# Causal mask moved from TensorE products into decay rows made by GpSimd, and parts of x prepared two slots earlier

## The chip, the cores and the metric

One core of a Trainium2 chip runs the whole kernel. The metric is the device time of one execution in microseconds (us). The engines are TensorE (PE in the profile, with its weight loads as PEld), VectorE (DVE), ScalarE (ACT), GpSimd (POOL) and SyncE (SP), which issues all the DMAs here.

## What is computed

Causal attention with a decay term, then a gated MLP, then a soft mixture of experts with 8 small experts. Cut to the part that the change touches:

```python
# q, k, v: (4, 8, 576, 64); f: (4, 8, 576)
scores = scale * q @ k.T
cum    = cumsum(log(clip(f, 1e-4, 1)))              # per batch and head
decay  = cum[:, None] - cum[None, :]
scores = where(upper triangle, -1e9, scores + decay)
attn   = softmax(scores)                            # row by row
out    = attn @ v                                   # 576 x 64 for each of 32 heads
# the 8 heads of a batch side by side are x (576 x 512), the input of the MLP:
h = x @ w_in;  g = h * sigmoid(1.702 * h);  x2 = g @ w_out
# then slots = softmax over tokens, 8 experts on 32 slots, and a mix back to the tokens
```

## The kernel before

The 32 heads are processed in order, n = 8 b + s for batch b and head s. Each head has five query tiles i = 0 to 4 (128 rows each, 64 in the last), and tile i needs only the keys up to its own diagonal block, 128 i + 128 columns (576 for tile 4). The kernel keeps the scores negated: TensorE makes -scale q k in `yb`, VectorE adds the row `cum` of the keys and takes the minimum along the row (L824, one instruction a tile, with a second one that reads the minimum out), ScalarE takes exp with scale -1 and that minimum as bias (L689). The causal mask is a constant `mask` of 128 x 128 that holds 1e9 above the diagonal. Before the change it is added by a matmul, identity times `mask_r`, into the diagonal block of each tile (L1059): five matmuls a head, 160 in all. `cum` is a row of 576 numbers, copied to all 128 partitions by one DMA a head (`load_cum`, L530) into `cum_b`, two heads deep.

Operands are kept as a high and a low part (fp32r). So ScalarE makes high parts (`qs`, `kh`, `pth`, `xh`, `gh`, `wih`, `woh`), VectorE or GpSimd the low parts. GpSimd's part of a head is `vsplit` (L626, L628) and `dup` (L615, L617), which copies the key parts to the other half of the partitions; TensorE's next scores wait for it. For x, ScalarE copies `xh` (L713) and GpSimd subtracts to `xl` (L633) for the pairs of heads 0 to 2; for pair 3, finished last, VectorE makes `xl` (L855).

The order of all engines' work is written out by `batch_steps`, which each engine's block walks with its own name. A slot is the stretch in which head s is scored and head s - 1 is turned, multiplied with v and summed. Batch 0 runs its attention alone ("begin" branch, slots 0 to 8; TensorE does 16 constant products, `fill`, L1082, in each slot). In batches 1 to 3 each slot also holds nine gaps, f(), into which the 64 units of the MLP of the batch before are spread. A unit is 12 matmuls of 288 columns (L1204); units alternate between two banks of `mb`, and a unit waits until the bank's last unit has been read. Eight units of the first kind (h, tanh on ScalarE L736, product on VectorE L925) alternate with eight of the second (into `x2t`, VectorE L932). The weights come quarter by quarter through a two-deep `stage` (L497), split by ScalarE (L675) and GpSimd (L660); GpSimd also makes `gl` (L643).

In the steps of a slot, VectorE's softmax normalisation (`norm`: L831, L833 and L838, one instruction for each of tiles 0 to 3; tile 4's is ScalarE's, L696) is followed by the first score tile of the next head ("early"). In slot 8, where the batch's last head is finished, the parts of x follow: on ScalarE `norm`, three xh copies (`early_x`), `pv` (L707, out of the attention's product), the fourth xh copy; on VectorE the sum of `pv` (L850) and the fourth xl. The first unit of the MLP waits for all four.

## Time and profile before

| | |
|---|---|
| median of 3 runs | 759.37 us (758.19 to 760.92) |
| the profiled execution's own time | 759.59 us |
| its span, first to last instruction | 757.8 us |
| TensorE busy | 712.0 us, 94% of the span, 6027 matmuls |
| VectorE, ScalarE, GpSimd busy | 58%, 58%, 53% |
| mean granted TensorE clock | 0.989 |
| chain that ended last | TensorE 78%, VectorE 10%, ScalarE 8%, issue 2% |
| HBM traffic | 126 GB/s over the span |

The span has four parts: batch 0's attention alone up to about 97 us, batches 1 to 3 with the MLP between (to about 566 us), the last batch's MLP (to about 685 us), and the mixture of experts. A matmul's duration in a row is its latency; matmuls overlap, so what one costs is read from the distance between starts. Rows of the same line that follow each other are merged, with their count behind an x.

### The profile page before, as it was taken

The page shows a single profiled execution, that of the slowest core. Times are in us where ns is not written, and L with a number is a line of the kernel's source. Part 1 is how long each engine was busy: PE and PEld are TensorE (multiplying, and loading weights), DVE is VectorE, ACT ScalarE, POOL GpSimd, SP SyncE. Part 2 cuts the span into 40 slices and gives each one's busy share as a digit, 9 for nine tenths or more (in the row PEclk, how much of TensorE's full clock was granted, in tenths as well). Part 3 has the DMA queues.
Part 4 walks back from the last instruction along what each step waited for, and adds up shares of the span by engine and source line. Part 5 has one row for each costly group of instructions (what it writes and reads, how often), then busy time and mean ns, then how long its engine had stood idle before and what let it go on. Part 6 is the DMA issues. An engine that isn't in the chain of part 4 may idle for free.

```text
span 757.8 us, 15776 instructions
## 1 busy us (share of the span) xinstructions
PE 712.0 (94%) x6027; PEld 678.2 (90%) x6027; DVE 443.0 (58%) x1255; ACT 435.9 (58%) x1031; POOL 399.5 (53%) x439
## 2 busy tenths in 40 slices
PE   3999979999999999999999999999999999998993
PEld 3888879999999999999999999999999999995562
DVE  6898857676776656675666566766542332225323
ACT  4788867575757675666666675757564344321113
POOL 3355357474747755565757573848385476530000
PEclk9999989999999999999999999999999999999998
DMA  4433323333333333333331413332214445499976
GB/s 105 107 93 107 93 67 89 89 89 88 96 95 96 96 84 94 85 106 85 107 85 48 133 37 95 95 108 68 70 44 139 139 141 193 136 394 376 380 301 250
DMA packets 90362, 96.65 MB, mean 128 GB/s; under 512 B 61296, under 2 KB 61296, under 8 KB 88240
## 3 DMA queue, kind: packets, MB, share of 16 engines
q1 hardware_dynamic: 90288, 95.66, 40.5%
q8 instruction: 48, 0.79, 0.4%
q14 instruction: 26, 0.21, 0.1%
HBM read 90.84 MB, written 4.79 MB: 126 GB/s over the span
## 4 chain that ended last, share of the span: by engine, by line
PE 78%; DVE 10%; ACT 8%; issue 2%; DMA 0%; POOL 0%; SPq 0%; DVEq 0%; POOLq 0%
PE mb L1204 51%; PE yb L1057 6%; PE zb L1076 5%; PE xb L1103 5%; PE mb L1256 2%; ACT prob L689 2%; DVE prob L838 2%; PE xb L1037 2%; DVE ptl L844 1%; ACT xh L713 1%; PE yb L1295 1%; PE yb L1059 1%; DVE kl L806 1%; DVE qs L802 1%; ACT qs L681 1%
## 5 line engine op out<-in xcount | busy, mean ns | idle before, releaser
L1204 PE MATMUL mb<-xh,wih 128*128 128x288 f32 x512 | 158.8, 310 | 7.4 <-DVE xl L855 4.3
L1204 PE MATMUL mb<-gh,woh 128*128 128x288 f32 x512 | 156.8, 306 | 3.1 <-DVE x2t L932 3.0
L1204 PE MATMUL mb<-xl,wih 128*128 128x288 f32 x512 | 151.5, 296 | 0.0
L1204 PE MATMUL mb<-xh,wil 128*128 128x288 f32 x512 | 151.3, 296 | 0.0
L1204 PE MATMUL mb<-gl,woh 128*128 128x288 f32 x512 | 150.8, 294 | 0.0
L1204 PE MATMUL mb<-gh,wol 128*128 128x288 f32 x512 | 150.8, 294 | 0.0
L643 POOL TENSOR_TENSOR gl<-hid,gh 128x288 fp32r<-128x288 f32 x128 | 105.1, 826 | 70.4 <-ACT gh L730 68.8
L925 DVE SCALAR_TENSOR_TENSOR hid<-gate,mb 128x288 f32<-128x288 f32 x128 | 57.6, 451 | 113.9 <-ACT gate L736 113.4
L689 ACT ACTIVATE prob<-prob,m_row 64x576 f32<-64x576 f32 (+4 forms) x160 | 96.5, 604 | 35.1 <-DVE m_row L824 34.2
L660 POOL TENSOR_TENSOR wol<-stage,woh 128x512 fp32r<-128x512 f32 x64 | 82.9, 1295 | 62.9 <-ACT woh L675 62.8
L660 POOL TENSOR_TENSOR wil<-stage,wih 128x512 fp32r<-128x512 f32 x64 | 82.1, 1291 | 56.9 <-ACT wih L675 56.7
L1204 PEld LDWEIGHTS mb<-xh,wih 128*128 128x128 f32 x512 | 96.9, 189 | 10.2 <-DVE hid L925 4.8
L736 ACT ACTIVATE gate<-mb 128x288 f32<-128x288 f32 x128 | 52.5, 410 | 83.8 <-PE mb L1204 83.1
L1204 PEld LDWEIGHTS mb<-gh,woh 128*128 128x128 f32 x512 | 96.3, 188 | 4.4 <-DVE x2t L932 3.9
L1204 PEld LDWEIGHTS mb<-xl,wih 128*128 128x128 f32 x512 | 97.1, 190 | 0.0
L1204 PEld LDWEIGHTS mb<-xh,wil 128*128 128x128 f32 x512 | 96.7, 189 | 0.0
L1204 PEld LDWEIGHTS mb<-gl,woh 128*128 128x128 f32 x512 | 96.3, 188 | 0.0
L1204 PEld LDWEIGHTS mb<-gh,wol 128*128 128x128 f32 x512 | 96.0, 188 | 0.0
L824 DVE CUSTOM_DVE_ANT_0 prob<-yb,cum_b 64x576 f32<-64x576 f32 (+4 forms) x160 | 83.5, 537 | 10.4 <-issue 9.8
L844 DVE TENSOR_TENSOR ptl<-zb,pth 128x512 fp32r<-128x512 f32 (+1 forms) x128 | 73.1, 571 | 24.4 <-ACT pth L702 23.8
L702 ACT CAST pth<-zb 128x512 fp32r<-128x512 f32 (+1 forms) x128 | 62.9, 491 | 41.7 <-PE zb L1076 41.1
L932 DVE SCALAR_TENSOR_TENSOR x2t<-mb,x2t 128x288 f32<-128x288 f32 x96 | 43.4, 454 | 71.2 <-PE mb L1204 71.0
(196 smaller groups left out, 1464.6 us busy)
## 6 DMA issues: line engine op xcount, KB each, us to landing
stage<-in_moe_w_in SPq DMA_DIRECT2D x64, 256.0 KB, 3.0
stage<-in_moe_w_out SPq DMA_DIRECT2D x64, 256.0 KB, 2.6
ring_a<-in_moe_w SPq DMA_DIRECT2D x16, 1024.0 KB, 6.7
ring_b<-in_moe_w SPq DMA_DIRECT2D x14, 1024.0 KB, 11.8
cum_b<-cum_dram SPq DMA_DIRECT2D x32, 288.0 KB, 3.7
qk_in<-in_q SPq DMA_DIRECT2D x32, 144.0 KB, 3.0
qk_in<-in_k SPq DMA_DIRECT2D x32, 144.0 KB, 3.7
v_in<-in_v SPq DMA_DIRECT2D x32, 128.0 KB, 3.2
```

The source lines that it names most:

```text
L643: pool.tensor_tensor(gl[:, i % FT, HALF * (i // FT):HALF * (i // FT + 1)], hid[:, i % RING, :], gh[:, i % FT, HALF * (i // FT):HALF * (i / ...
L660: pool.tensor_tensor(lo[:, t, :], stage[:, t % 2, :], hi[:, t, :].bitcast(F32), ALU.subtract).then_inc(w_lo, 1)
L689: nc.scalar.activation(prob[0:r, par, POFF[i]:POFF[i] + w], prob[0:r, par, POFF[i]:POFF[i] + w], ACT.Exp, bias=m_row[0:r, par, i:i + 1], s ...
L702: nc.scalar.copy(pth[:, lo:hi], zb[:, c % 2, 0:hi - lo]).then_inc(p_hi, 1)
L736: nc.scalar.activation(gate[:, j % RING, :], bank_of("unit", m, u)[:, 0:HALF], ACT.Tanh, scale=GATE / 2).then_inc(h_tanh, 1)
L824: nc.vector.tensor_tensor_reduce(prob[0:r, par, o:o + w], ybf[0:r, base:base + w], cum_b[0:r, par, 0:w], 1.0, 3e38, ALU.add, ALU.min, m_ro ...
L844: nc.vector.tensor_tensor(ptl[:, lo:hi], zb[:, c % 2, 0:hi - lo], pth[:, lo:hi].bitcast(F32), ALU.subtract).then_inc(p_lo, 1)
L925: nc.vector.scalar_tensor_tensor(out=hid[:, j % RING, :], in0=gate[:, j % RING, :], scalar=1.0, in1=bank[:, 0:HALF], op0=ALU.add, op1=ALU. ...
L932: nc.vector.scalar_tensor_tensor(out=dst, in0=bank[:, 0:HALF], scalar=0.5, in1=dst, op0=ALU.mult, op1=ALU.add).then_inc(unit_out, 1)
L1057: mm(ybf[:, base + k0:base + k0 + kw], qs[:, par, P * i:P * i + P], x[:, par, k0:k0 + kw], start=not last, stop=last, skip_group_check=True)
L1076: ins = tr(zb[:, c % 2, at:at + P], prob[:, par, POFF[i] + P * kt:POFF[i] + P * kt + P], swapped if back else ident)
L1204: ins = mm(bank[:, 0:HALF], a[:, t, P * (j % 4):P * (j % 4) + P], x[:, t, cols], start=(i == 0), stop=(i == 11))
```

## The change

Four things:

1. For batches 1 to 3 the mask matmul is gone. The decay row is instead loaded once for each query tile (`COFF`: where each tile's copy begins in 1856 columns), so that each has a diagonal block of its own, and GpSimd adds `mask` to those blocks: 64 x 64 for tile 4 (`cmask_4`, behind `dup`), and two instructions of two 128 x 128 blocks each for the others (`cmask`). `cmask` waits for `normed`, VectorE's normalisation of the head before. Even heads use free space in `x2tok`, odd heads the place of the old `cum_b`.
2. SyncE issues five DMAs of cum a head instead of one; four of them (tiles 3, 2, 0, 1) go behind the loads of v, q and k of the same slot.
3. In batch 0 the parts of x's pairs 0 and 1 are made in slot 7, that of pair 2 in slot 8. On ScalarE pairs 0 and 2 stand at the slot's beginning and pair 1 ahead of `norm`; on GpSimd pairs 0 and 2 stand behind `vsplit` and pair 1 behind `cmask`. In later batches `early_x` is as it was.
4. TensorE does 16 constant products ahead of the first unit of batch 0's MLP.

```diff
+CW = 1856
+COFF = [512, 1024, 640, 0, 1280]
@@ batch_steps
         if engine == "pool":
-            qk, dup = qk + dup, []
+            qk, dup = qk + dup + following_head("cmask_4"), []
+            early = following_head("cmask")
@@
+        first_x = [[(1, ("xsplit", kt))] if begin and engine in ("act", "pool") and slot == at_slot else []
+                   for kt, at_slot in enumerate((HEADS - 1, HEADS - 1, HEADS))]
@@ begin branch
+            if engine == "act":
+                steps += first_x[0] + first_x[2]
@@
-                          + norm + early_x + pv + xs[3])
+                          + first_x[1] + norm + pv + xs[3])
             else:
-                steps += (vsplit + pt(0) + score(1) + pt(1) + score(2) + qk + pt(2) + score(3) + dup + pt(3)
-                          + norm + early + early_x + pv + xs[3])
+                steps += (vsplit + pt(0) + score(1) + first_x[0] + first_x[2] + pt(1) + score(2) + qk + pt(2) + score(3) + dup + pt(3)
+                          + norm + early + first_x[1] + pv + xs[3])
@@ SyncE, load_cum (first in a slot's load) and load_cum_tiles (last in it)
+                sp.dma_start(cum_t[s % 2][0:QW[4], COFF[4]:CW], cum_dram[bass.ds(n, 1), :].to_broadcast([QW[4], SEQ])
+                             ).then_inc(c_dma_4[s % 2], 16)
+                for i in (3, 2, 0, 1) if n >= HEADS else ():
+                    w = P * i + QW[i]
+                    sp.dma_start(cum_t[s % 2][:, COFF[i]:COFF[i] + w], cum_dram[bass.ds(n, 1), 0:w].to_broadcast([P, w])
+                                 ).then_inc(c_dma[s % 2], 16)
@@ GpSimd
+                elif st[0] == "cmask_4":
+                        pool.wait_ge(c_dma_4[n % 2], 16 * (n // 2 - 3))
+                        pool.tensor_tensor(at, at, mask[0:QW[4], 0:QW[4]], ALU.add).then_inc(c_masked_4, 1)
+                elif st[0] == "cmask":
+                        pool.wait_ge(c_dma[n % 2], cum_loaded(n))
+                        pool.wait_ge(normed, n)
+                        for at in (blocks[:, 0:5:4, :], blocks[:, 1:7:5, :]):
+                            pool.tensor_tensor(at, at, mask[:, :].unsqueeze(1).broadcast_to([P, 2, P]), ALU.add
+                                               ).then_inc(c_masked, 1)
@@ VectorE, score
+                        if b:
+                            dve.wait_ge(c_masked_4, b * 8 + s - HEADS + 1)
+                    elif g < 3 and b:
+                        dve.wait_ge(c_masked, 2 * (b * 8 + s - HEADS) + g)
@@ TensorE, score
-                        ins = mm(ybf[:, base + P * i:base + P * i + r], ident_r[:, :], mask_r[:, 0:r],
-                                 start=False, stop=True, skip_group_check=True)
+                        if b == 0:
+                            ins = mm(ybf[:, base + P * i:base + P * i + r], ident_r[:, :], mask_r[:, 0:r],
+                                     start=False, stop=True, skip_group_check=True)
@@ TensorE, unit
+                    if b == 1 and st[1] == 0 and m == 0:
+                        constant_products()
```

## Rows read from the trace of the kernel before

**Rows 1.** Windows view, busy time of each engine in the three middle batches

```profile
core 0: us, PE busy (x) PEld busy (x) DVE busy (x) ACT busy (x) POOL busy (x), PEclk, DMA share, GB/s
105.40:260.00 154.60, 150.92 (x1167) 149.10 (x1167) 106.44 (x285) 101.64 (x244) 99.49 (x108) 1.00 0.33 90
260.00:420.00 160.00, 157.92 (x1251) 155.53 (x1250) 101.61 (x296) 105.24 (x253) 99.47 (x109) 1.00 0.33 91
420.00:566.00 146.00, 145.27 (x1148) 142.98 (x1146) 88.06 (x254) 94.38 (x227) 87.58 (x94) 1.00 0.28 79
```

**Rows 2.** Chain that ended last, from 105 to 566 us, shares by line

```profile
by line: PE mb L1204 59.0%; PE yb L1057 8.2%; PE zb L1076 7.5%; PE xb L1103 7.3%; PE xb L1037 1.9%; ACT xh L713 1.6%; PE yb L1059 1.5%; DVE prob L838 1.3%; ACT gate L736 1.1%; issue 1.0%; ACT gh L730 1.0%; DVE hid L925 0.9%; ACT prob L689 0
```

**Rows 3.** Timeline of TensorE, matmuls with idle time before them: start, duration, [idle <-releaser]

```profile
101.02 0.61 PE L1204 MATMUL mb<-xh,wih 128*128 128x288 f32 x1 [4.28 <-DVE xl L855]
...
121.78 0.40 PE L1204 MATMUL mb<-xh,wih 128*128 128x288 f32 x1 [1.40 <-DVE hid L925]
...
153.73 0.40 PE L1204 MATMUL mb<-xh,wih 128*128 128x288 f32 x1 [0.83 <-DVE hid L925]
...
252.28 0.40 PE L1204 MATMUL mb<-gh,woh 128*128 128x288 f32 x1 [1.36 <-DVE x2t L932]
...
566.40 0.40 PE L1204 MATMUL mb<-gh,woh 128*128 128x288 f32 x1 [0.25 <-DVE x2t L932]
```

**Rows 4.** Timeline of TensorE: 16 constant products, and one mask matmul among scores

```profile
81.70 1.98 PE L1082 MATMUL mb<-mask_r,ident_r 128*128 128x128 f32 x16
...
298.64 0.22 PE L1059 MATMUL yb<-mask_r,ident_r 128*128 128x128 f32 x1
298.70 0.39 PE L1057 MATMUL yb<-kh,qs 128*128 128x384 f32 x1
298.93 0.34 PE L1057 MATMUL yb<-kl,qs 128*128 128x384 f32 x1
```

**Rows 5.** Timeline at the end of batch 0's last slot

```profile
94.15 0.37 PE L1057 MATMUL yb<-kh,qs 128*128 128x288 f32 x1
...
95.41 0.28 PE L1103 MATMUL xb<-ptl,vs 128*128 128x64 f32 x1
95.43 1.80 ACT L713 CAST xh<-xst 128x576 fp32r<-128x576 f32 x3
...
96.23 4.11 POOL L633 TENSOR_TENSOR xl<-xst,xh 128x576 fp32r<-128x576 f32 x3 [2.18 <-ACT xh L713]
...
97.26 0.63 ACT L707 COPY olow<-xb 64x576 f32<-64x576 f32 x1
...
99.41 1.55 DVE L855 TENSOR_TENSOR xl<-xst,xh 128x576 fp32r<-128x576 f32 x1 [0.74 <-ACT xh L713]
```

**Rows 6.** Timeline of the same slot: ScalarE at its beginning, GpSimd's dup

```profile
87.69 0.59 ACT L702 CAST pth<-zb 128x512 fp32r<-128x512 f32 x1 [0.26 <-PE zb L1076]
...
91.81 1.14 POOL L615 TENSOR_TENSOR kh<-kh,mask 64x576 fp32r<-64x576 f32 x1 [2.55 <-ACT kh L683]
```

**Rows 7.** Windows view behind TensorE's long idle time (columns as in rows 1)

```profile
103.00:105.00 2.00, 2.00 (x12) 1.99 (x10) 0.25 (x1) 0.70 (x2) 0.00 (x0) 0.50 0.00 0
```

**Rows 8.** Groups of instructions, GpSimd: busy us, mean ns of one

```profile
L643 POOL TENSOR_TENSOR gl<-hid,gh 128x288 fp32r<-128x288 f32 x128 | 105.1, 826 | 70.4 <-ACT gh L730 68.8
```

**Rows 9.** Groups of VectorE, one normalisation tile at 208.1 and at 94.5 us

```profile
L838 DVE TENSOR_SCALAR prob<-prob,rsum 128x384 f32<-128x384 f32 x1 | 1.4, 1443 | 0.0
...
L838 DVE TENSOR_SCALAR prob<-prob,rsum 128x384 f32<-128x384 f32 x1 | 0.4, 415 | 0.0
```

**Rows 10.** Timeline at the end of batch 1's last slot

```profile
246.99 4.20 POOL L633 TENSOR_TENSOR xl<-xst,xh 128x576 fp32r<-128x576 f32 x3 [1.71 <-ACT xh L713]
...
251.10 0.76 DVE L855 TENSOR_TENSOR xl<-xst,xh 128x576 fp32r<-128x576 f32 x1 [0.74 <-ACT xh L713]
...
251.78 0.81 DVE L932 SCALAR_TENSOR_TENSOR x2t<-mb,x2t 128x288 f32<-128x288 f32 x2
```

**Rows 11.** Timeline of SyncE's queue, the one cum load of a head

```profile
255.40 0.43 SPq L530 DMA_DIRECT2D cum_b<-cum_dram  x1
```

More of the change, by code:

```diff
@@ L292, in build @@
         v_in = sb("v_in", [P, 2, QT, DIM], F32, att_mem)
-        cum_b = sb("cum_b", [P, 2, SEQ], F32, att_mem)
+        cum_1 = sb("cum_1", [P, CW], F32, att_mem)
+        cum_b = cum_1[:, 0:2 * SEQ].rearrange("p (x n) -> p x n", x=2)
+        cum_t = (x2tok[:, 2 * QT:3 * QT, :].rearrange("p i n -> p (i n)")[:, 0:CW], cum_1[:, :])
         qs = sb("qs", [P, 2, QT * P], F32R, att_mem)
@@ L372, in build @@
         c_dma = [sem(f"c_dma{i}") for i in range(2)]
+        c_dma_4 = [sem(f"c_dma_4{i}") for i in range(2)]
+        c_masked = sem("c_masked")
+        c_masked_4 = sem("c_masked_4")
         w_dma = [sem(f"w_dma{i}") for i in range(2)]
@@ L463, in bank_of, with cum_loaded @@
             return mb[:, place[kind, m, i] % 2, :]
+        def cum_loaded(n):
+            return 16 * (n // 2 + 1) if n < HEADS else 64 + 16 * (QT - 1) * (n // 2 - 3)
         def is_last(m):
@@ L528, in load_cum, with load_cum_tiles @@
                 wait_from(sp, decayed, 5 * (n - 1))
-                src = cum_dram[bass.ds(n, 1), :].to_broadcast([P, SEQ])
-                sp.dma_start(cum_b[:, s % 2, :], src).then_inc(c_dma[s % 2], 16)
+                if n < HEADS:
+                    sp.dma_start(cum_b[:, s % 2, :], cum_dram[bass.ds(n, 1), :].to_broadcast([P, SEQ])
+                                 ).then_inc(c_dma[s % 2], 16)
+                    return
+                sp.dma_start(cum_t[s % 2][0:QW[4], COFF[4]:CW], cum_dram[bass.ds(n, 1), :].to_broadcast([QW[4], SEQ])
+                             ).then_inc(c_dma_4[s % 2], 16)
+            def load_cum_tiles(b, s):
+                n = b * 8 + s
+                for i in (3, 2, 0, 1) if n >= HEADS else ():
+                    w = P * i + QW[i]
+                    sp.dma_start(cum_t[s % 2][:, COFF[i]:COFF[i] + w], cum_dram[bass.ds(n, 1), 0:w].to_broadcast([P, w])
+                                 ).then_inc(c_dma[s % 2], 16)
             def step(b, m, st):
@@ L538, in step @@
                         load_qk((n + 1) // HEADS, (n + 1) % HEADS)
+                    load_cum_tiles(b, st[1])
                 elif st[0] == "weights":
@@ L618, in step @@
                     pool.wait_ge(k_dup, 2 * n + 2)
+                elif st[0] == "cmask_4":
+                    n = b * 8 + st[1]
+                    if n >= HEADS:
+                        pool.wait_ge(c_dma_4[n % 2], 16 * (n // 2 - 3))
+                        at = cum_t[n % 2][0:QW[4], COFF[4] + 4 * P:CW]
+                        pool.tensor_tensor(at, at, mask[0:QW[4], 0:QW[4]], ALU.add).then_inc(c_masked_4, 1)
+                elif st[0] == "cmask":
+                    n = b * 8 + st[1]
+                    if n >= HEADS:
+                        pool.wait_ge(c_dma[n % 2], cum_loaded(n))
+                        pool.wait_ge(normed, n)
+                        blocks = cum_t[n % 2][:, P * 3:P * 10].rearrange("p (x n) -> p x n", n=P)
+                        for at in (blocks[:, 0:5:4, :], blocks[:, 1:7:5, :]):
+                            pool.tensor_tensor(at, at, mask[:, :].unsqueeze(1).broadcast_to([P, 2, P]), ALU.add
+                                               ).then_inc(c_masked, 1)
                 elif st[0] == "vsplit":
@@ L1026, in _, with constant_products @@
             pe.wait_ge(phi_in, 16)
+            def constant_products():
+                for _ in range(FILL):
+                    mm(mb[:, 0, 0:P], ident_r[:, :], mask_r[:, :], start=True, stop=True)
             def step(b, m, st):
@@ L1056, in step @@
                             for x, last in ((kh, False), (kl, True)):
-                                mm(ybf[:, base + k0:base + k0 + kw], qs[:, par, P * i:P * i + P],
-                                   x[:, par, k0:k0 + kw], start=not last, stop=last, skip_group_check=True)
-                        ins = mm(ybf[:, base + P * i:base + P * i + r], ident_r[:, :], mask_r[:, 0:r],
-                                 start=False, stop=True, skip_group_check=True)
+                                ins = mm(ybf[:, base + k0:base + k0 + kw], qs[:, par, P * i:P * i + P],
+                                         x[:, par, k0:k0 + kw], start=not last, stop=last, skip_group_check=True)
+                        if b == 0:
+                            ins = mm(ybf[:, base + P * i:base + P * i + r], ident_r[:, :], mask_r[:, 0:r],
+                                     start=False, stop=True, skip_group_check=True)
                     ins.then_inc(scored, 1)
@@ L1080, in step @@
                 elif st[0] == "fill":
-                    for _ in range(FILL):
-                        mm(mb[:, 0, 0:P], ident_r[:, :], mask_r[:, :], start=True, stop=True)
+                    constant_products()
                 elif st[0] in ("pv_first", "pv"):
@@ L1134, in step @@
                 elif st[0] == "unit":
+                    if b == 1 and st[1] == 0 and m == 0:
+                        constant_products()
                     unit(b, m, st[1])
```

6 lines of the change are left out of this document (4 added, 2 removed).

## Prediction

> **What bounds the kernel now.** I read the windows view first. In the three middle batches TensorE is busy for 150.92 of 154.60, 157.92 of 160.00 and 145.27 of 146.00 us, at the full clock (level 1.00, 2.4 GHz), while VectorE, ScalarE and GpSimd have 60 to 69% [rows 1]. The reader is to see that this stretch, 461 us of 757.8, is paced by TensorE's own stream, so that a matmul taken out of it is worth its issue distance. The chain of waits says the same: its TensorE lines add up to 85.4% there, and about 14% runs over other engines [rows 2]. In those parts a shorter TensorE stream only waits longer. The timeline then shows where TensorE really stands still: 1.40 and 0.83 us for VectorE's product in batch 1, 1.36 us at the end of the batch's last slot (the next batch has the same wait at the same place; the third only 0.25), and, far the longest, 4.28 us before the first MLP unit, for VectorE's low part of x's fourth pair [rows 3].
>
> **Part 1, 120 mask matmuls gone.** 24 heads by 5. What is one worth? Two rows bound it. Sixteen identical products in a row take 1.98 us from the first start to the last end; taking off one latency of about 0.28, the 15 steps are 0.11 us each [rows 4]. Among scores, the mask matmul starts at 298.64 and the next one at 298.70, only 0.06 later; but the one after that starts at 298.93, 0.23 behind its 384-column predecessor, because its weight load could not hide behind the short matmul. The 384 columns themselves need 0.16 at 2.4 GHz, and a long matmul behind a long one starts after that; the other 0.06 or so is the mask matmul's doing. So 0.06 + 0.06 = 0.12 goes with this one. I take 0.109, the constant product, which is the same instruction: 120 x 0.109 = **13.1 us**. Ends: 0.06 gives 7.2, 0.12 gives 14.4. Of the 13.1, 14% lies where the chain runs over other engines [rows 2]: **-1.8 us**.
>
> The Trainium skill (TensorE: Matmul & The Clock Gate, section "Back-to-back issue gap") gives about 81 ns as the sustained distance of load and matmul pairs of 128 columns. By it this term would be an estimated 9.7 us instead of 13.1, and the time about 752, between the forecast and rival (c); the rows here give 109 ns, and I go by them.
>
> **Part 2, GpSimd's new work.** No row shows a 2 x 128-column add with a broadcast mask. The nearest is `gl`, 288 columns in 826 ns [rows 8]; by columns 256 cost 0.73, two of them 1.5 us, and the 64 x 64 block at most 0.35. So 1.8 us a head on an engine that is idle for over 7 of its 19 to 20 us a slot [rows 1]. Beside TensorE this costs nothing in itself. What it can cost is the clash with VectorE. A normalisation tile of 384 columns takes 415 ns alone and 1443 ns when GpSimd's instructions run back to back beside it [rows 9]; so a VectorE instruction that works between SBUF operands stands until GpSimd's instruction ends. The SBUF page of the Trainium skill (SBUF — State Buffer, section "SBUF: two separate sides") says that the pair of ports shared by VectorE and GpSimd is locked for the whole instruction; it speaks against this change, and the row agrees. Standing behind `normed`, the two adds miss the normalisation; VectorE's next work (first score tile, products, sums out of PSUM) showed no such stretching in the rows I read. `cmask_4` pushes GpSimd's queue 0.35 later just ahead of the normalisation, and `cmask` another 1.5 behind it; queued behind are `gl` and the weight splits, on which ScalarE's gate (four buffers deep) and the stage loads hang. Cover for that is three units of 1.6 us; I charge **-1.0 us** over 24 heads for the times when it fails (0 to 4).
>
> One place is not random: the last slot of batches 1 to 3. There GpSimd makes three xl parts, now behind `cmask`. Before, they ran from 246.99 to 251.19, and VectorE's own xl at 251.10 took 0.76 undisturbed [rows 10]. Now they start some 1.4 us later and run to 252.6, so VectorE's xl arrives between two of them and may wait for up to 1.4, as it did at 99.41, where it took 1.55 beside the last of three [rows 5]. Behind it in VectorE's queue is the read of `x2t` at 251.78, and for that TensorE already waits [rows 3, 10]. I take 0.8 for this and 0.2 for the 0.35 us and the later weight splits: **-3.0 us** for three batches (0 to 4.5).
>
> **Part 3, SyncE and DMA.** Five issues instead of one, at 0.43 plus gap: 1.9 us more a head [rows 11]. Behind them on the queue are the stage loads; in the slots I read, the stage load that follows a head's loads is used 7 to 12 us later, and those used at once are issued before them, so nothing is due. v, q and k go ahead of four of the five. The bytes rise from 288 KB to 0.8 MB a head, on DMA engines that are 28 to 33% busy [rows 1]. **0**; if a stage load were hit, up to 1.9 us in a slot.
>
> **Part 4, the junction of batch 0 and 1.** Before: three xh copies (1.80 us) stand between `norm` and `pv` on ScalarE, so olow starts at 97.26 although its product was ready at about 95.7 (last matmul at 95.41, latency 0.28); later VectorE's xl takes 1.55 instead of 0.76 because of GpSimd's third xl [rows 5, 10]. Alone these two are 1.5 + 0.8 = 2.3 us. But the moved work costs something. ScalarE is nearly full in these slots: a copy of 0.6 to 0.67 at the beginning finds 0.26 us of idle time, so it delays the slot by about 0.4 [rows 6], somewhat less (0.2) in slot 7; pair 1 finds a wait of VectorE's reciprocal and costs nothing. On GpSimd slot 7's end now holds `cmask` (1.5) and xl of pair 1 (1.4) and slot 8 another xl, before the `dup` that started at 91.81 after 2.55 us of idling: 4.3 us more against gaps of 2.55 here and about as much before vsplit, the latter opening for `cmask` only when the normalisation ends. Worked through, dup starts at 93.0 instead of 91.81; its end lets TensorE start the early scores, then at 94.15, now at 95.3 [rows 5, 6]. From there: product ready 96.8, olow to 97.4, sum to 98.2, xh to 98.9, xl (undisturbed) to 99.7. The unit starts at 99.7 instead of 101.02: **+1.3 us** (0 to 2.3).
>
> **Part 5, 16 constant products there.** They take 1.7 to 2.0 us right behind the first turn, while TensorE would wait until 99.7 anyway: cost 0 as long as the wait is over 2 us; without it up to 2.0. Before, after 4.28 us of standing still, the clock was at 0.50 (1.2 GHz) and the units ran at 0.24 us a matmul [rows 3, 7] instead of 0.13; up to about 105.4 this lost 1.4 us in the first unit and 0.5 in five turns. With under 1 us of idle time left I expect the clock to stay at 1.00: **+1.9 us** (0 to 1.9).
>
> **Sum.** 13.1 - 1.8 - 1.0 - 3.0 + 1.3 + 1.9 = 10.5 us. The profiled execution took 759.6 us, 1.8 more than its span and 0.2 over the median, so 759.6 - 10.5 = 749.1, and against the median **749.0 us**.
>
> **Rivals.**
> (a) More comes back. Today's two stalls of batch 1 (1.40 and 0.83) hang on a contended normalisation; batch 2, in another phase, has neither. If the new phase spares them and the last slots lose only 0.3 each: 749.0 - 2.2 - 2.1 = 744.7. For it: parked at `cmask`, GpSimd is quieter near VectorE. Against: those clashes come from work ahead of `cmask`.
> (b) Cover fails. A shorter TensorE stream meets the read-out of the banks more often; twice the lost share (another 1.8) and the full 4.5 at the last slots and 2 more elsewhere: 749.0 + 5.3 = 754.3. The 14% of the chain on other engines speaks for it.
> (c) A mask matmul is worth only the 0.06 to the next start: 749.0 + 5.1 = 754.1 (less the lost share of it). The 0.23 behind it speaks against.
> (d) The clock falls all the same, because early scores are later still: 749.0 + 1.9 = 750.9, and with part 4 at 0, 752.2; that part 4 moves the wait rather than removing it is the case in which the change doesn't do what it says.
> (e) Slower than before, by one mechanism at one place: GpSimd, late by `cmask`, runs into the next normalisation in every head, and one more tile stands 1.03 us (1443 - 415). That is 24.7 us on VectorE; in place of my -4.0 it gives 749.0 - 4.0 + 24.7 = 769.7. It decides from 0.6 us a head on. Against it are 7 us of idling a slot.
>
> **How the numbers follow.** Forecast 0.47 (746 to 752), (a) 0.20, (b) 0.13, (c) 0.07, (d) 0.08, (e) with its milder forms 0.05. The range from 743.5 to 755 takes in (a) to (d) and leaves out (e) and the outer ends. A difference of 0.3% (2.3 us, 757.1 to 761.6) is about what a measurement of this kernel can tell from no change: faster 0.94, same 0.03, slower 0.03.
>
> **What would show it.** In the changed profile L1059 has 40 instances; TensorE's first unit starts near 99.7 at clock 1.00; the middle batch's period, about 160 us [rows 1], shrinks by 3 to 4 us; the stall at the last slot's end grows by about 1 us, with L855 over 1 us. If mean L838 rises, (e) is right; if TensorE shows new waits for L925 or L932 in mid batch, (b); if `cmask` instances take far more than 0.75 us, part 2 is mis-sized.

## The result, and the profile after

The changed kernel takes 757.27 us (median of 10 runs, 754.74 to 758.0) beside 760.69 for the kernel before (10 runs, 758.19 to 763.64): ratio 0.9949, 95% interval 0.9936 to 0.9963. It is faster by about 0.5%, but of the 10.5 us forecast only 3.4 to 3.9 came, and the time lies outside the range. The profiled execution took 757.33 us, its span is 755.5.

The windows view of the kernel after, busy time of each engine in the middle batches (the stretches and columns of [rows 1]):

```profile
105.40:260.00 154.60, 146.83 (x1115) 144.43 (x1114) 110.00 (x284) 98.87 (x239) 109.29 (x130) 0.99 0.48 112
260.00:420.00 160.00, 155.07 (x1217) 152.03 (x1216) 102.42 (x298) 107.55 (x255) 113.65 (x133) 1.00 0.47 118
420.00:566.00 146.00, 143.60 (x1125) 140.62 (x1124) 89.70 (x255) 94.16 (x226) 100.17 (x114) 1.00 0.42 101
```

TensorE's idle time grew in each window: 3.7 to 7.8 us, 2.1 to 4.9, and 0.7 to 2.4. GpSimd's busy time grew by 10 to 14 us a window, as planned. VectorE's grew by 3.6 us in the first, although the change gives it nothing to do.

The timeline of TensorE after, the matmuls behind waits over 0.5 us from the first unit on (start, duration, ..., [idle <-releaser]); [rows 3] answers to it:

```profile
100.04 0.40 PE L1260 MATMUL mb<-xh,wih 128*128 128x288 f32 x1 [0.56 <-DVE xl L905]
...
118.76 0.40 PE L1260 MATMUL mb<-xh,wih 128*128 128x288 f32 x1 [1.99 <-DVE hid L975]
...
151.35 0.40 PE L1260 MATMUL mb<-xh,wih 128*128 128x288 f32 x1 [0.94 <-DVE hid L975]
...
192.79 0.40 PE L1260 MATMUL mb<-xh,wih 128*128 128x288 f32 x1 [1.13 <-DVE hid L975]
...
211.70 0.40 PE L1260 MATMUL mb<-gh,woh 128*128 128x288 f32 x1 [1.33 <-DVE x2t L982]
...
251.18 0.40 PE L1260 MATMUL mb<-gh,woh 128*128 128x288 f32 x1 [1.84 <-DVE x2t L982]
...
264.63 0.40 PE L1260 MATMUL mb<-xh,wih 128*128 128x288 f32 x1 [2.19 <-DVE x2t L982]
...
410.00 0.40 PE L1260 MATMUL mb<-gh,woh 128*128 128x288 f32 x1 [1.84 <-DVE x2t L982]
...
422.49 0.40 PE L1260 MATMUL mb<-xh,wih 128*128 128x288 f32 x1 [1.25 <-DVE x2t L982]
```

The 4.28 us wait is now 0.56 (the 16 constant products fill part of the difference). Four new waits stand in mid batch or just behind the last slot (192.79, 211.70, 264.63, 422.49), and the old ones at 121.78, 252.28 and 412.02 are longer by 0.5 to 0.6. Adding up all waits over 0.16 us from behind the first unit to the end of batch 3's attention gives 6.42 us before and 14.55 after: **8.1 us of new standing still**.

The first of these has a second price. The windows view behind it (clock is the first number behind the counts):

```profile
118.00:122.00 4.00, 3.24 (x17) 3.23 (x18) 1.56 (x5) 1.89 (x5) 2.77 (x5) 0.74 0.88 234
122.00:126.00 4.00, 4.00 (x26) 3.91 (x26) 1.80 (x6) 2.78 (x6) 3.01 (x4) 0.84 0.46 86
```

At the junction, where it had been at 0.57 (98 to 106 us before), the clock stays at 1.00. Here it is partly at its lower level: 4 x 0.26 + 4 x 0.16 = 1.7 us given back.

The account of the profiled executions closes with this. First unit to the mark at the end of batch 3's attention ([rows 3], 101.02 to 566.40): 465.38 us before, 462.45 after (100.04 to 562.49). Masks -10.8 (measured below), waits +8.1, clock at the junction -1.9, clock at 120 us +1.7: -2.9, as measured. The 1.9 is the forecast's own estimate. Measured on x_only below, it is 2.1: from the first unit to the wait near 120 us it takes 17.24 us, the kernel before 19.36, for the same matmuls. With 2.1 the sum is -3.1. With the first unit 0.98 earlier, the mark is 3.9 us earlier. Behind it, where nothing was changed, this execution lost 1.6 us (the clock was lower for longer at 690 to 702 us), so that the spans differ by 2.3; the medians differ by 3.4.

### The profile page after: what moved, and what is told of

It reads as the page before. It is cut to its first block, busy times and chain, and to the rows that moved or that the text cites. A ratio compares the mean times of both kernels' runs of the same rounds, so it can differ in the third digit from the quotient of the medians.

```text
span 755.5 us, 15808 instructions
## 1 busy us (share of the span) xinstructions
PE 703.7 (93%) x5923; PEld 666.7 (88%) x5923; DVE 448.8 (59%) x1255; ACT 436.8 (58%) x1031; POOL 438.6 (58%) x511
## 4 chain that ended last, share of the span: by engine, by line
PE 71%; DVE 12%; ACT 7%; issue 3%; POOL 3%; DMA 1%; SPq 0%; DVEq 0%; POOLq 0%
PE mb L1260 47%; PE yb L1111 5%; PE zb L1131 5%; PE xb L1157 4%; PE mb L1312 2%; DVE prob L888 2%; ACT prob L733 2%; DVE sums_e L881 2%; DVE ptl L894 2%; PE xb L1091 2%; PE yb L1351 1%; POOL xl L677 1%; DMA stage<-in_moe_w_in 1%; DVE kl L850 1%; DVE qs L846 1%
## 5 line engine op out<-in xcount | busy, mean ns | idle before, releaser
L687 POOL TENSOR_TENSOR gl<-hid,gh 128x288 fp32r<-128x288 f32 x128 | 103.2, 811 | 36.1 <-ACT gh L774 35.3
L975 DVE SCALAR_TENSOR_TENSOR hid<-gate,mb 128x288 f32<-128x288 f32 x128 | 57.7, 451 | 107.7 <-ACT gate L780 107.2
L982 DVE SCALAR_TENSOR_TENSOR x2t<-mb,x2t 128x288 f32<-128x288 f32 x96 | 43.4, 454 | 66.0 <-PE mb L1260 65.8
L1131 PE MATMUL zb<-ident,prob 128*128 128x128 f32 x480 | 73.6, 278 | 2.9 <-DVE prob L888 2.8
```

The source lines that it names most:

```text
L687: pool.tensor_tensor(gl[:, i % FT, HALF * (i // FT):HALF * (i // FT + 1)], hid[:, i % RING, :], gh[:, i % FT, HALF * (i // FT):HALF * (i / ...
L975: nc.vector.scalar_tensor_tensor(out=hid[:, j % RING, :], in0=gate[:, j % RING, :], scalar=1.0, in1=bank[:, 0:HALF], op0=ALU.add, op1=ALU. ...
L982: nc.vector.scalar_tensor_tensor(out=dst, in0=bank[:, 0:HALF], scalar=0.5, in1=dst, op0=ALU.mult, op1=ALU.add).then_inc(unit_out, 1)
L1131: ins = tr(zb[:, c % 2, at:at + P], prob[:, par, POFF[i] + P * kt:POFF[i] + P * kt + P], swapped if back else ident)
```

## Experiments

Ratios are against the kernel before on the same chip, with 95% intervals; the medians of before in these comparisons were 760.42 us (before_no_mask, no_adds, x_only, mask_only), 761.13 (only_4, late_cmask, no_normed, mid_cmask) and 760.98 (the three repairs). A difference between two kernels of different groups carries the error of both ratios. Line numbers in the rows are each kernel's own and can differ by one or a few for the same instruction.

### before_no_mask: what the mask matmuls are worth

The kernel before, with the mask matmuls of batches 1 to 3 left out and nothing in their place (these blocks stay unmasked).

```diff
-                        ins = mm(ybf[:, base + P * i:base + P * i + r], ident_r[:, :], mask_r[:, 0:r],
-                                 start=False, stop=True, skip_group_check=True)
+                        if b == 0:
+                            ins = mm(... the same ...)
```

> The kernel before, with the 120 mask matmuls of batches 1 to 3 simply left out (so the diagonal blocks of these batches are not masked; no masks in the decay rows, no new DMAs, no parts of x moved). Theory G (GpSimd's new work, not TensorE's saving, is what failed): TensorE's stream alone is worth about 11 us, ratio to before about 0.986, stalls of TensorE in the middle batches about 6 to 8 us in total as before. Rival S (a shorter stream of TensorE meets the other engines by itself): ratio about 0.994, with stalls near 14 us as in the changed kernel. Rival D (the new DMAs are the cost) expects the same as G here.

Measured: 751.26 us, ratio 0.9880 (0.9856 to 0.9905). In the trace, first unit to the mark went from 465.38 to 455.72 us, -9.66, while the waits went from 6.42 to 7.61. So the stream itself lost 9.66 + 1.2 = 10.8 us, **0.090 us a matmul**, and little of it was eaten by waits. (Behind its first unit the clock is low for 5.4 us, against 4.6 before, which is worth another 0.4 us and would make it 0.094.) So rival S, a shorter stream that meets the other engines by itself, is out.

### no_adds and only_4: GpSimd's adds

The kernel after, in which each add writes one column instead (same waits, same DMAs, almost no time on GpSimd; the mask is left out). only_4 does this to the two big adds alone and keeps the small one.

```diff
-                        pool.tensor_tensor(at, at, mask[0:QW[4], 0:QW[4]], ALU.add).then_inc(c_masked_4, 1)
+                        pool.memset(at[:, 0:1], 0.0).then_inc(c_masked_4, 1)
...
-                            pool.tensor_tensor(at, at, mask[:, :].unsqueeze(1).broadcast_to([P, 2, P]), ALU.add
-                                               ).then_inc(c_masked, 1)
+                            pool.memset(at[:, :, 0:1], 0.0).then_inc(c_masked, 1)
```

> The changed kernel with GpSimd's three adds a head replaced by one-column memsets that signal the same semaphores (so the diagonal blocks of batches 1 to 3 are not masked and one column of each is cleared); DMAs, waits and order unchanged. Theory G: the stalls of VectorE's row-sum and normalisation instructions and the late weight splits go, ratio to before 0.984 to 0.986 (about 748). Rival D (DMAs: stage loads land 0.9 us later, masks wait for their rows): stays near 0.995. Rival S: stays near 0.995.

> The changed kernel with the two large adds a head (cmask, 1.43 us) replaced by one-column memsets, the small one (cmask_4, 0.31 us, right ahead of the normalisation's place) kept; so the diagonal blocks of tiles 0 to 3 of batches 1 to 3 are not masked. If it is the large adds behind the normalisation that make GpSimd late (theory L), this is as without all adds: ratio to before 0.984 to 0.986. If it is the small add, which pushes the other work 0.3 us further into VectorE's row sum (rival E), 0.990 or more stays lost.

Measured: no_adds 748.51 us, ratio 0.9838 (0.9821 to 0.9854), TensorE's waits 7.53 us. That is near the forecast's 749.0, but without the adds, for which the forecast had charged 4.0 us. Rival D, that the new DMAs are the cost, is out by the same run. The adds cost 1.1% of the time, some 8.4 us, and the five DMAs and their issues cost nothing that shows. only_4: 753.27 us, ratio 0.9903 (0.9875 to 0.9931). So the small adds, 24 instructions of 0.31 us, 7.6 us in all on an engine that idles 40% of the time, cost 0.65%, **4.9 us** (by the intervals 2 to 7); the 48 big ones, 34 us of work, 3.5 (1 to 6). Which of the two is the larger the intervals leave open. What they do show is that the cost doesn't go with the amount of work: four and a half times the work cost no clearly larger time. The traces say the same: from the first unit to the mark it is 453.41 us in no_adds, 459.56 in only_4 and 462.45 after, and the waits are 7.53, 11.82 and 14.55. The rest of the first step is the clock. no_adds has no fall in this stretch, only_4 has one, behind a wait of 1.86 us at 249.58, and the kernel after has one, at 120 us, so that up to 1.7 us of the small add's cost is a fall, and none of the big ones'.

### What the small add does

The groups of VectorE (busy us, mean ns | idle before) in the kernel before:

```profile
L838 DVE TENSOR_SCALAR prob<-prob,rsum 128x128 f32<-128x128 f32 (+3 forms) x128 | 52.8, 475 | 1.1
L831 DVE TENSOR_SCALAR sums_e<-sums 128x5 f32<-128x5 f32 x32 | 9.7, 304 | 7.6 <-ACT prob L689 7.6
```

in the kernel after:

```profile
L888 DVE TENSOR_SCALAR prob<-prob,rsum 128x128 f32<-128x128 f32 (+3 forms) x128 | 45.8, 421 | 1.1
L881 DVE TENSOR_SCALAR sums_e<-sums 128x5 f32<-128x5 f32 x32 | 23.8, 743 | 7.9 <-ACT prob L733 7.9
```

and in only_4:

```profile
L880 DVE TENSOR_SCALAR sums_e<-sums 128x5 f32<-128x5 f32 x32 | 23.5, 734 | 7.7 <-ACT prob L732 7.7
```

The reader is to see that the row sum, the smallest instruction of the softmax, 5 columns, has become 2.4 times as long on average with the small add alone; the normalisation is shorter in exchange, since the clash is over when it begins. VectorE loses 14.1 and gets back 7.0. The loss is not spread evenly: 9.8 of the 14.1 us come from four heads of batch 1, at 113.34, 132.73, 188.01 and 206.15. One instance shows how. VectorE and GpSimd before, head 5 of batch 1:

```profile
205.79 1.14 POOL L617 TENSOR_TENSOR kl<-kl,mask 64x576 fp32r<-64x576 f32 x1
...
207.01 1.60 POOL L643 TENSOR_TENSOR gl<-hid,gh 128x288 fp32r<-128x288 f32 x2
...
207.78 0.17 DVE L831 TENSOR_SCALAR sums_e<-sums 128x5 f32<-128x5 f32 x1
...
208.21 3.57 DVE L838 TENSOR_SCALAR prob<-prob,rsum 128x128 f32<-128x128 f32 x4
```

and after:

```profile
204.16 1.14 POOL L646 TENSOR_TENSOR kl<-kl,mask 64x576 fp32r<-64x576 f32 x1
...
205.38 0.32 POOL L653 TENSOR_TENSOR cum<-cum,mask 64x64 f32<-64x64 f32 x1
...
205.66 1.56 POOL L687 TENSOR_TENSOR gl<-hid,gh 128x288 fp32r<-128x288 f32 x2
...
206.15 3.60 DVE L881 TENSOR_SCALAR sums_e<-sums 128x5 f32<-128x5 f32 x1
207.19 2.53 POOL L704 TENSOR_TENSOR wil<-stage,wih 128x512 fp32r<-128x512 f32 x2
...
210.00 1.27 DVE L888 TENSOR_SCALAR prob<-prob,rsum 128x128 f32<-128x128 f32 x4
```

In both the row sum comes 0.85 us behind the end of `dup`. Before, that is the moment at which the first of two `gl` ends (207.01 + 0.80) and the second begins, and the sum takes 0.17 us. After, the add has pushed `gl` by 0.28 us; the sum arrives in its middle and stands until the last of four back-to-back GpSimd instructions ends (207.19 + 2.53 = 209.72; 206.15 + 3.60 = 209.75). Sum and normalisation together take 5.1 us instead of 4.0, and behind them waits the read of `x2t`, which TensorE needs at 211.70: the new 1.33 us wait. At 113.34, 188.01 and 132.73 the sum took 2.78, 2.83 and 2.33 us, and the first two stand ahead of the 1.99 and 1.13 us waits; each time the sum ended 0.03 us behind the last of two or three GpSimd instructions that followed each other. The clock's fall at 120 us stands behind such a wait too. Before, and in no_adds, small_ahead, x_only and before_no_mask (waits of 1.40, 1.07, 1.02, 1.40 and 1.58 at this place), there is none; in mask_only (1.97) there is; in late_cmask (1.98) and only_4 (1.97) there isn't. So at this place a fall was seen only behind the longer wait, and not behind each of them.

### x_only and mask_only: the two halves apart

x_only is the kernel before with part 3 of the change and the 16 constant products; mask_only is the kernel after without them.

```diff
-                          + norm + early_x + pv + xs[3])
+                          + first_x[1] + norm + pv + xs[3])
...
+                        for _ in range(FILL):
+                            mm(mb[:, 0, 0:P], ident_r[:, :], mask_r[:, :], start=True, stop=True)
```

> The kernel before with the x part alone: first three pairs in batch 0's last two slots, and 16 constant products before the first unit; masks by matmul as before. Without cmask on GpSimd the first unit should start at about 99.3 us instead of 101.0 with the clock at 1.00, which is worth 1.7 + 1.9 = 3.6 us if nothing gives it back: ratio 0.995. If the next stalls and a later clock fall take it back, as the changed kernel's clock at 0.50 around 120 us suggests, ratio 0.998 to 1.000.

> The changed kernel without the x part: first three pairs made at the end of slot 8 of batch 0 as before, no constant products. If the two parts add, this is the changed kernel's 0.995 plus what the x part gives (0.2 to 0.5%): 0.997 to 0.999. Under rival S and under G alike; it tells what of the changed kernel's 3.8 us is the masks' part.

Measured: x_only 759.85 us, ratio 0.9991 (0.9975 to 1.0006); mask_only 761.70, ratio 1.0003 (0.9989 to 1.0017). The mask part alone gains nothing; the two halves together gain 0.5%. They need each other, and the reason is at the junction. In mask_only `cmask` pushes all three of GpSimd's xl parts there, as it does in the last slots of the other batches, and TensorE's first unit says so:

```profile
103.52 0.61 PE L1258 MATMUL mb<-xh,wih 128*128 128x288 f32 x1 [5.53 <-POOL xl L677]
```

From slot 7's first turn to this unit it is 24.49 us, against 23.23 before, 21.96 after and 22.60 in x_only; and the clock is at 0.59 from 102 to 110 us, so the 1.9 us of part 5 are lost too. Its trace has two more falls, behind waits of 1.97 us at 124.53 and 1.99 at 415.64, where the kernel after has one. x_only in its turn falls short of the forecast 1.3 by 0.7: GpSimd's xl of pair 1 runs beside VectorE's normalisation there, which takes 2.43 us instead of 1.27, and TensorE's turns wait 1.39 us for it (L842, at 89.16). In the kernel after `cmask` stands between them, behind `normed`, and this wait is 0.35 us (87.48).

### late_cmask: the big adds out of the way in the last slots

In slot 8 of batches 1 to 3, GpSimd makes x's low parts first and the two big adds behind them.

```diff
-                      + qk + f() + score(3) + pt(3) + dup + f() + norm + f() + early
-                      + (early_x + f() + pv + xs[3] if s == 0 else f()) + f(2))
+                      + qk + f() + score(3) + pt(3) + dup + f() + norm + f() + (early if engine != "pool" or s else [])
+                      + (early_x + f() + pv + xs[3] if s == 0 else f()) + (early if engine == "pool" and s == 0 else []) + f(2))
```

> The changed kernel with one move: in the last slot of batches 1 to 3 GpSimd makes x's three low parts first and adds the masks behind them. Theory X (there the adds push the low parts, these the weight splits, these the next stage load, and ScalarE waits 1.5 to 5.5 us for it): TensorE's waits of 2.19 us at 264.6 and 1.25 us at 422.5 go, ratio 0.990 to 0.992. Rival D2 (the stage load lands late because of the added DMAs, 4.6 us instead of 3.8): the waits stay at over half of that and the ratio at 0.994.

The reason to try it is the chain of waits of the kernel after behind the end of batch 1's last slot, in order of time (start, us, what):

```profile
245.89 1.44 POOL cum L661 x2
247.33 4.70 POOL xl L677 x3
252.03 0.76 POOL gl L687
252.80 2.50 POOL wil L704 x2
255.29 0.02 issue
255.31 4.64 DMA stage<-in_moe_w_in
259.95 0.02 issue
259.98 0.62 ACT wih L719
260.60 0.72 ACT prob L733 x2
261.32 0.48 ACT pth L746
```

and so on over VectorE's `ptl`, `qs` and `kl` to its read of `x2t` at 264.12, for which TensorE waited 2.19 us. This is the queue that the prediction named and then costed at almost nothing: `cmask`, the three xl (4.70 us instead of the 4.20 of [rows 10]; the last of them stood for VectorE's own xl and ran from 250.04 to 252.03), the weight split, the stage load, ScalarE's high part, and behind that ScalarE's `pth` for the attention.

Measured: 756.57 us, ratio 0.9944 (0.9925 to 0.9962), no better than the change itself. Yet the waits behind the last slots are gone (264.6) or down to 0.40 (422.5), and the sum of the waits is 11.44 instead of 14.55 us. What took it back is in the windows view of this kernel (clock first behind the counts):

```profile
250.00:258.00 8.00, 7.63 (x44) 7.52 (x45) 3.49 (x9) 2.15 (x5) 6.83 (x8) 0.79 0.39 101
406.00:414.00 8.00, 6.16 (x36) 5.86 (x35) 3.03 (x7) 3.65 (x7) 6.89 (x7) 0.79 0.17 47
```

0.21 x 16 = up to 3.4 us lost at the lower clock level, behind the two 1.84 us waits for VectorE at 250.37 and 408.33. The kernel after has these two waits with the same length and no fall behind them, and its fall at 120 us is in turn absent here, so that the difference is 1.7 us. Waits -3.1 and clock +1.7 give -1.4, and the stretch from the first unit to the mark is 460.91 us instead of 462.45. Of these 1.5 us, 0.75 had been lost ahead of the first unit in this execution, where the two kernels are the same, and the medians tell no difference. Theory X is right as to the waits, then, and its 0.990 to 0.992 was not reached; rival D2, for which they would have stayed, is out. Why the clock falls at the one place and not at the other is not settled.

### no_normed and mid_cmask: other places for the adds

no_normed lets GpSimd add as soon as the rows have landed, without waiting for the normalisation; mid_cmask does all three adds ahead of `dup`.

```diff
-                        pool.wait_ge(normed, n)
```

```diff
-            qk, dup = qk + dup + following_head("cmask_4"), []
-            early = following_head("cmask")
+            qk, dup = following_head("cmask_4") + following_head("cmask") + qk + dup, []
+            early = []
...
-                        pool.wait_ge(normed, n)
```

> The changed kernel without GpSimd's wait for VectorE's normalisation (no data hangs on it; the adds then start as soon as the rows are there). If the wait does its work (theory W), the adds now run beside the row sum and the normalisation, whose groups grow by up to 1.4 us a head, and the ratio goes to 1.000 or above. If the wait itself is the cost (rival P: GpSimd stands 1.7 us in front of it and starts its own work late), the ratio falls to 0.988 to 0.991.

> The changed kernel with all three adds ahead of the copies of the keys (dup), in the middle of the slot before the one that uses them, where GpSimd stood idle waiting for ScalarE's keys (51.7 us in 32 heads in the kernel before), and without the wait for the normalisation. Theory G says place, not amount, decides: most of the lost 8 us returns, ratio 0.986 to 0.989. Rival A (GpSimd's total work is what VectorE meets): as the changed kernel, 0.995; and if dup now comes late for the scores, 1.000.

Measured: no_normed 772.43 us, ratio 1.0160 (1.0128 to 1.0192). The row sum's mean is 950 ns, the normalisation's 489 instead of 421, and TensorE's waits add up to 23.5 us, 8.9 more than after. The clock falls three times in mid batch (0.79 in 118 to 126 us and in 198 to 206, 0.72 in 218 to 230), 5.1 us of time more than after. Over the kernel after, the medians are 2.1% apart, which the wait for `normed` saves. It is a mechanism like that of rival (e), an add that runs into VectorE's softmax. That the time is near the 769.7 us given there is luck: VectorE's two groups grew by 15.4 us over the kernel after, not 24.7, and the row sum took a good part of it.

mid_cmask: 851.92 us, ratio 1.1205 (1.1165 to 1.1245), where 0.986 to 0.989 had been expected. The row sum is short here (290 ns, while the normalisation has 590), but the place stops the kernel in another way. Its view of waits (engine, line, releaser: us in total, times, longest):

```profile
PE yb L1110 <- issue: 57.4, 14, 6.4
POOL x2tok L660 <- DMA x2tok<-cum_dram: 56.0, 10, 9.5
POOL cum L660 <- DMA cum<-cum_dram: 37.9, 9, 6.3
```

GpSimd, at the add, waits for rows that SyncE issues behind stage loads; these wait for GpSimd's own weight splits (SyncE waited for them 107 times, for up to 17.9 us), which stand behind the add. With `dup` behind it too, TensorE's early scores wait for the whole round. The same adds in this place cost 91 us over the kernel before; part of that is the clock, whose mean is 0.937.

### small_ahead, both_moved and both_hold: repairs

small_ahead puts the small add ahead of `dup`, both_moved adds the edit of late_cmask. both_hold adds to that 8 constant products in batches 1 and 2, ahead of the unit that waits at the end of the last slot.

```diff
-            qk, dup = qk + dup + following_head("cmask_4"), []
+            qk, dup = qk + following_head("cmask_4") + dup, []
```

```diff
+                    if st[1] == HELD and m < BATCH - 2:
+                        pe.wait_ge(p_lo, 32 * (m + 2))
+                        for _ in range(8):
+                            mm(zb[:, 1, 0:P], ident_r[:, :], mask_r[:, :], start=True, stop=True, skip_group_check=True)
```

> The changed kernel with one move: GpSimd's small add (tile 4, 0.31 us) stands ahead of the copies of the keys instead of behind them. Its rows have landed 5 us or more before in every slot of the changed kernel's trace, and there GpSimd waited for ScalarE's keys 0.2 to 5.7 us. Theory E (the small add, by pushing GpSimd's queue into VectorE's row sum, costs about 5 us): where the idle time there is over 0.3 us it goes, so batch 1's waits of 1.99, 1.13 and 1.33 us shrink, ratio to before 0.990 to 0.992. Rival N (its place among the copies makes no difference, since at batch 2 and 3 GpSimd idles only 0.2 us there): 0.994 to 0.996.

> Both moves: the small add ahead of the copies of the keys, and in the last slot of batches 1 to 3 the large adds behind x's low parts. If the two losses are separate and nothing takes their place, 0.985 to 0.989. If TensorE's clock falls again at the waits of 1.84 us at the end of batches 1 and 2, as it did with the second move alone (0.71 and 0.86 there), up to 3.5 us stay lost: 0.990 to 0.992.

> As the kernel with both moves, and TensorE does 8 constant products (0.9 us, into a bank of zb that is free then) inside its wait at the end of batches 1 and 2, ahead of the unit that ended the 1.84 us of idle time. If the fall of the clock behind that wait is a cost of its own (theory C, about 1.7 us each time it falls), the granted clock stays at 1.00 around 250 and 408 us and the median is 1 to 3.5 us below that of both moves. If the clock falls for another reason, no difference.

| kernel | median us | ratio (95%) | row sum, mean ns | TensorE's waits, us |
|---|---|---|---|---|
| after | 757.27 | 0.9949 (0.9936 to 0.9963) | 743 | 14.55 |
| small_ahead | 752.01 | 0.9879 (0.9858 to 0.9899) | 355 | 10.85 |
| both_moved | 750.78 | 0.9864 (0.9849 to 0.9879) | 355 | 10.33 |
| both_hold | 750.75 | 0.9862 (0.9848 to 0.9876) | 316 | 7.84 |
| no_adds | 748.51 | 0.9838 (0.9821 to 0.9854) | 332 | 7.53 |

The waits of both_hold would be 1.7 us more if its constant products were counted as waiting. small_ahead does the same work with two steps swapped, and is 0.7% faster than the change, more than the 0.990 expected of it. Its groups of VectorE:

```profile
L888 DVE TENSOR_SCALAR prob<-prob,rsum 128x128 f32<-128x128 f32 (+3 forms) x128 | 52.3, 471 | 1.1
L881 DVE TENSOR_SCALAR sums_e<-sums 128x5 f32<-128x5 f32 x32 | 11.4, 355 | 7.9 <-ACT prob L733 7.9
```

They are back at the values of before (52.8 and 9.7), and its waits at 192.79 and 211.70 are gone; the one at 118 is 1.02 us, without a fall of the clock. Two comparisons now agree on the small add's part: 5.3 us by this run (3 to 7 by the intervals), 4.9 by only_4 against no_adds. both_moved and both_hold mask every block and are the fastest such kernels of this study, 1.4% under the kernel before. Their intervals overlap each other and that of small_ahead, so that the second move and the constant products are not shown to add anything. In both_hold's trace TensorE's timeline at the last slot's end and behind it reads

```profile
245.53 0.40 PE L1264 MATMUL mb<-gh,woh 128*128 128x288 f32 x1 [0.72 <-DVE x2t L982]
...
257.94 0.40 PE L1264 MATMUL mb<-xh,wih 128*128 128x288 f32 x1 [1.15 <-DVE x2t L982]
```

against 1.56 and 1.77 us in both_moved. The 8 products fill 0.84 of the 1.56 and gain nothing by it; both_moved's own trace has the clock at 1.00 behind these waits, so there was nothing to hold. Whether they help in executions in which the clock does fall is open. both_hold's four runs spread over 2.0 us (749.22 to 751.18), both_moved's five over 4.2 (750.27 to 754.46), but that speaks for nothing: the 754.46 is the traced one, whose clock held behind these waits and was low far behind them (0.63 in 686 to 700 us, against 1.00 in both_hold), where the kernels don't differ.

## Why the prediction was wrong, point by point

**What bounds the kernel: right.** 120 matmuls taken out of TensorE's stream gave 9.1 us of median with nothing put in their place (before_no_mask). That part of the forecast stood.

The account against the 10.5 us: without the adds the sum was 14.5 and no_adds measured 12.3, the 2.2 being part 1's (11.3 forecast net, 9.1 measured); the adds took 8.4 instead of 4.0. 10.5 - 2.2 - 4.4 = 3.9, which is the ratio's 0.51%. These are differences of medians with errors of 1 to 2 us each, so that the exact agreement is partly luck.

**Part 1: mechanism right, term too big.** I took 0.109 us a mask, from a run of identical constant products; the stream gave 0.090. 120 x 0.019 = 2.3 us too much. The row itself gives (1.98 - 0.28) / 15 = 0.113, so that 0.109 does not follow from it, and "the same instruction" was wrong for one mask in five: that of tile 4 has 64 columns, not 128. How much of the difference this makes was not measured. Rival (c)'s 0.06 was too little: the matmul behind a mask was indeed late by its weight load. The Trainium skill (TensorE: Matmul & The Clock Gate, section "Back-to-back issue gap"), with about 81 ns, was nearer than my row, though under the measured 90. The lost share on other engines was 1.2 us by before_no_mask, with 1.8 forecast. (The sum at the end has a slip of 0.1: against the median of 759.37 the forecast is 748.9.)

**Part 2: the step that failed.** The durations were right: the big adds took 0.735 us each (0.73 forecast) and the small one 0.315 (at most 0.35). Wrong was what they do to others. I charged 1.0 us for GpSimd's lateness in mid batch and 3.0 at the last slots; TensorE's waits with the adds are 7.0 us longer than without (14.55 against 7.53), and by the medians the adds cost 8.4 us instead of 4.0. The fall of the clock, 1.7 us, which no_adds hasn't, makes up the rest. Two readings were at fault. First, "standing behind `normed`, the two adds miss the normalisation" was said of `cmask` and was right (no_normed shows what it saves), but for `cmask_4` I looked only at what is queued behind it, `gl` and the splits, and not at what VectorE would be doing when these came 0.28 us later. I watched L838, while the instruction that came to stand was the row sum ahead of it, L831 (L881 after), which had taken 0.17 us at 207.78 and seemed too small to matter. The rule that I quoted (SBUF — State Buffer, section "SBUF: two separate sides") is borne out (3.60 us instead of 0.17), with the addition that two to four GpSimd instructions went through ahead of VectorE's one.

Second, at the last slots I placed the loss on VectorE's own xl (0.8 of my 1.0 each). That clash came the other way round: L905 took 0.76 us at 250.00 and at 408.82, and at 250.04 GpSimd's third xl stood for it, 1.99 us instead of 1.42. The loss came by the path that I had costed at 0.2: `cmask`, xl, weight split, stage load, ScalarE, 2.19 us at 264.63 and 1.25 at 422.49. The stage load took 4.64 us to land there, with the median at 3.0 us before and 3.7 after. The median is 3.6 in no_adds too, so that it comes with the new cum loads and not with the adds; by itself it cost nothing that shows there.

**Part 3: right in the sum.** no_adds has all the new DMAs and issues and is the fastest kernel of all.

**Part 4: right by 0.03 us.** 1.3 forecast, 1.27 measured from slot 7's first turn to the first unit. The steps came too: `dup` at 93.22 (93.0), the early scores at 95.57 (95.3), the unit at 100.04 (99.7), with the turn itself 0.29 later than before. An agreement to 0.03 is luck. What I had not seen is that it depends on part 2: with x's parts alone it is 0.63, and without them the adds cost 1.26 there.

**Part 5: right at its place, and taken back 20 us later.** The clock stayed at 1.00 at the junction and gave the 1.9 us (2.1 by x_only); the 1.99 us wait at 118.76 lost 1.7 of them. I had written rival (d) for a fall at the junction only.

**The rivals.** The outcome is (b), cover fails, and beyond its size (5.3 us over the forecast; it came to 8.3 by the medians, and to 6.6 against the kernel before of the same chip), by a clash of (e)'s kind, though not of its pair: the small add with the row sum, and not `cmask` with the normalisation. Of the signs named, those for (b) came true: new waits for the reads of `hid` and `x2t` in mid batch (L975, L982). Two signs of the forecast itself failed: the middle batch's period shrank by 0.9 us (from 252.28 to 412.02 before, from 251.18 to 410.00 after) and not by 3 to 4, and the stall at the last slot's end grew by 0.5 us without L905 rising over 1. The sign for (e), a rising mean of the normalisation, spoke the wrong way: it fell from 475 to 421 ns because the row sum took the clash in its place. Whoever looked at that line alone would have read an improvement. Of (a), nothing came.

**The range** was too narrow on the upper side because I bounded each term by itself. I had bounded GpSimd's lateness over 24 heads by 0 to 4 us as if it were a matter of chance; but the order of two steps is the same in every head, and where the phase is bad it does harm each time: in four of eight heads of batch 1 the row sum took over 2 us, in batches 2 and 3 never more than 1.33. And a fall of the clock in mid batch, behind a wait that grows to some 1.9 us from the 1.40 of before, was in no term.

## What to carry to other kernels

Before adding an instruction to an engine that shares SBUF with VectorE, look at the whole run of instructions that it pushes, and ask which VectorE instruction, however small, will now arrive in the middle of it instead of at a boundary: here 0.3 us of work a head cost some 5 us of time over 24 heads, and swapping two steps got it back. When an engine off the critical path is loaded further at the end of a stage, follow its queue through the loads that it frees up to the engine that bounds; the wait ended 19 us behind the start of its cause (245.89 to 264.63). And judge a change of two parts by both halves alone and by a version that keeps all the waits and transfers but none of the work: this showed at once that the mask was worth moving, and two steps swapped then got back most of what the adds had cost.

## What the runs showed of the hardware

- VectorE's row sum of 5 columns took 0.17 us when it arrived at the boundary of two GpSimd instructions (207.78 before) and 3.60 us when it arrived inside one, until a run of four back-to-back GpSimd instructions was over (206.15 after). It did not get in between them; at 113.34, 132.73 and 188.01 it stood over three, two and three. Other VectorE instructions did get in at a boundary: the low part of x arrived at 250.00, 0.07 us ahead of one, took 0.76 us, and the GpSimd instruction behind the boundary stood instead, 1.99 us instead of 1.42. What decides between the two is not settled.
- The granted clock fell behind the same wait early in batch 1 where it was 1.99 us (after) and 1.97 (mask_only), not where it was 1.98 (late_cmask), 1.97 (only_4), or 1.02 to 1.58 (before, no_adds, before_no_mask, small_ahead, x_only, both_moved, both_hold). 1.84 us near 251 had a fall behind it in late_cmask and none in after, and 1.86 at 249.58 had one in only_4 and at 407.54 none; 2.19 at 264.63 in after had none, and 2.21 at 417.78 in small_ahead had one. The length of the wait alone doesn't decide it; what else does, these runs don't settle.
- A mask matmul (four of 128 columns and one of 64 in a head) between the scores' matmuls of 128 to 512 columns was worth 0.090 us on average, less than the distance of 0.113 in a row of identical ones of 128 columns.
